# Tile 0's P is transposed at place 7 of a pair, in front of the other pair's second P V group

## The reference, cut to what matters

```
scale = 1.0 / np.sqrt(q.shape[-1])
scores = scale * np.matmul(q, k.transpose(0, 1, 3, 2))       # 4 x 8 heads, 576 x 576, depth 64
thresh = np.max(scores, axis=-1, keepdims=True) - tau
scores = np.where(scores >= thresh, scores, -1000000000.0)
scores = scores - np.max(scores, axis=-1, keepdims=True)
attn = np.exp(scores)
attn = attn / (np.sum(attn, axis=-1, keepdims=True) + 1e-09)
x = np.matmul(attn, v)                                       # -> 2304 tokens x 512
...
h = x @ w_in;  r = np.maximum(h, 0.0);  x = (s * (r * r) + b) @ w_out
...
h = x @ w_in2; x = (np.maximum(h, 0.0) + alpha * np.minimum(h, 0.0)) @ w_out2
```

## Time and profile before

| what | value |
| --- | --- |
| time, median of 3 runs | 1088.46 us (1088.38 to 1089.14) |
| time of the profiled execution | 1089.1 us |
| its span | 1087.3 us |
| TensorE busy | 99% of the span |
| VectorE, ScalarE, GpSimd busy | 48%, 47%, 24% of the span |
| mean granted TensorE clock | 0.996 of full speed |
| one pair in the steady part of attention | 17.34 us |

### The profile page before, as it was taken

One profiled execution on the slowest core, in us unless ns is written; L12 is line 12 of the kernel. 1 busy time (PEld: TensorE's weight loads), 2 busy tenths in 40 slices (PEclk: granted clock), 3 DMA queues, 4 the chain that ended last, 5 costly groups with the idle time before them and its releaser, 6 DMA issues.

```text
span 1087.3 us, 18967 instructions
## 1 busy us (share of the span) xinstructions
PE 1075.3 (99%) x5826; PEld 892.6 (82%) x5826; DVE 526.4 (48%) x1017; ACT 505.9 (47%) x946; POOL 257.3 (24%) x438
## 2 busy tenths in 40 slices
PE   8999999999999999999999999999999999999998
PEld 7877877777788888888888889888888888888897
DVE  7988989888643332242242246522422332332232
ACT  4877878787754332232232235544433333333343
POOL 3666656666574200000000014322000000000000
PEclk8999999999999999999999999999999999999999
DMA  8666666565121100000000003211100100010010
GB/s 187 159 148 160 153 143 157 139 152 135 40 58 49 49 1 1 1 0 0 0 0 0 0 20 88 87 49 30 40 0 0 39 0 0 0 39 0 0 39 20
DMA packets 86554, 59.28 MB, mean 55 GB/s; under 512 B 49376, under 2 KB 69872, under 8 KB 86512
## 3 DMA queue, kind: packets, MB, share of 16 engines
q1 hardware_dynamic: 83248, 57.58, 20.6%
q10 hardware_dynamic: 3264, 1.18, 0.5%
HBM read 30.94 MB, written 4.72 MB: 33 GB/s over the span
## 4 chain that ended last, share of the span: by engine, by line
PE 91%; ACT 3%; DVE 2%; issue 2%; SPq 1%; DMA 0%; ACTq 0%; DVEq 0%
PE psum L947 23%; PE psum L948 23%; PE psum L949 23%; PE psum L1084 6%; PE psum L1050 5%; PE psum L976 3%; PE psum L978 3%; DVE act_r L883 2%; PE psum L1079 1%; ACT pt L645 1%; PE psum L960 1%; PE psum L1058 1%; ACT ex L623 1%; ACT win_hi L600 1%; SPq L434 1%
## 5 line engine op out<-in xcount | busy, mean ns | idle before, releaser
L947 PE MATMUL psum<-x_hi,win_hi 128*128 128x512 f32 (+1 forms) x640 | 235.7, 368 | 0.0
L948 PE MATMUL psum<-x_lo,win_hi 128*128 128x512 f32 (+1 forms) x640 | 235.5, 368 | 0.0
L949 PE MATMUL psum<-x_hi,win_lo 128*128 128x512 f32 (+1 forms) x640 | 235.5, 368 | 0.0
L947 PEld LDWEIGHTS psum<-x_hi,win_hi 128*128 128x128 f32 x640 | 120.7, 189 | 20.8 <-DVE x_lo L876 0.2
L948 PEld LDWEIGHTS psum<-x_lo,win_hi 128*128 128x128 f32 x640 | 120.6, 188 | 20.4
L949 PEld LDWEIGHTS psum<-x_hi,win_lo 128*128 128x128 f32 x640 | 120.7, 189 | 19.9
L894 DVE SCALAR_TENSOR_TENSOR act_r<-act_n,nalpha,act_r 128x512 f32<-128x512 f32 (+1 forms) x80 | 56.1, 702 | 155.6 <-ACT act_r L724 155.4
L883 DVE SCALAR_TENSOR_TENSOR act_r<-act_r,s_c 128x512 f32<-128x512 f32 (+1 forms) x80 | 73.1, 914 | 111.0 <-ACT act_r L713 111.0
L716 ACT ACTIVATE g_hi<-act_r,b_c 128x512 fp32r<-128x512 f32 (+1 forms) x80 | 54.5, 681 | 151.7 <-PE psum L949 121.6
L557 POOL TENSOR_SCALAR ex<-ex,none_in,rinv 128x576 f32<-128x576 f32 x142 | 117.1, 827 | 30.0 <-DVE rinv L814 29.2
L623 ACT ACTIVATE ex<-psum,negm 128x576 f32<-128x576 f32 x144 | 107.1, 747 | 29.2 <-DVE negm L795 28.1
(11 more groups left out here) (94 smaller groups left out, 1611.2 us busy)
## 6 DMA issues: line engine op xcount, KB each, us to landing
k_twice<-k_hi SPq DMA_DIRECT2D x64, 144.0 KB, 2.4
stage<-in_moe_w_out_dram SPq DMA_DIRECT2D x32, 256.0 KB, 2.6
out_dram<-stage SPq DMA_DIRECT2D x18, 256.0 KB, 2.2
q_both<-q_hi SPq DMA_DIRECT2D x32, 128.0 KB, 2.3
q_both<-q_lo SPq DMA_DIRECT2D x32, 128.0 KB, 2.3
win_raw<-in_moe_w_in_dram SPq DMA_DIRECT2D x16, 256.0 KB, 2.9
stage<-in_moe_w_in_dram SPq DMA_DIRECT2D x16, 256.0 KB, 2.7
raw_q<-in_q_dram SPq DMA_DIRECT2D x30, 128.0 KB, 2.4
```

The source lines that it names most:

```text
L947: nc.tensor.matmul(dst, lhs[0], rhs[0], start=first, stop=False)
L948: nc.tensor.matmul(dst, lhs[0], rhs[1], start=False, stop=False)
L949: return nc.tensor.matmul(dst, lhs[1], rhs[0], start=False, stop=final)
```

## The change

Turn 0 goes from place 8 to place 7 in the table. At place 8 it stood behind the other pair's second P V group and behind the fill of tile 7; now it stands in front of both.

```
@@ -212,7 +212,7 @@
-        TURNS = [(8, 0, False), (9, 1, False), (10, 2, False), (10, 3, False), (11, 0, True),
+        TURNS = [(7, 0, False), (9, 1, False), (10, 2, False), (10, 3, False), (11, 0, True),
                  (11, 4, False), (12, 5, False), (13, 6, False), (13, 7, False), (16, 4, True)]
```

## The result

| kernel | median us | lowest to highest | runs | span of the profiled execution | its own time |
|---|---|---|---|---|---|
| before | 1088.78 | 1087.92 to 1089.43 | 20 | 1087.3 | 1089.10 |
| changed | 1090.26 | 1089.91 to 1092.12 | 20 | 1088.6 | 1090.37 |

The ratio is 1.0017, with an interval of 1.0011 to 1.0023: 0.17% slower, inside the band of 0.2% that was forecast as the likeliest, and inside the range; the upper end of the interval lies outside the band. It is nevertheless a real loss of some 1.8 us where 0.0 was worked out, and the trace says where it lies.

A forecast was written before the change was run, and what follows sets the result against it. The prediction took a ring over four engines, no single one, as the bound. +0.3 us over 15 pairs and -0.3 in pair 0 summed to 0.0, giving a median of 1088.5 us, range 1086.2 to 1091.0.

The forecast's parts named there:

- the band of 0.2%: Whole kernel: time within 0.2% (2.2 us) of before, about what a measurement can tell from no change; chance 0.63.
- +0.3 - 0.3 = 0.0: Whole kernel, in us: +0.02 a pair over 15 pairs, less 0.3 gained in pair 0, leaves the time unchanged.
- Turn 1's wait: TensorE behind the fill of tile 8: the wait for ScalarE's copy of group 1 goes, freeing 0.14 us.
- Turn 0's slot: TensorE between the fill of tile 6 and P V: four transposes take 0.44 us, bounds 0.35 and 0.50.
- VectorE and ScalarE: Steady pair: tile 7's maximum 0.44 us later, tile 8's 0.23 later, ScalarE's exponential of tile 8 0.07 earlier.
- The mask of tile 8: VectorE: start set by the latest of ScalarE 165.16, VectorE 165.27, GpSimd 165.25, against 165.23; +0.02 us a pair taken.
- the ring: Chain of waits over four engines, from tile 7's fill through tile 8's mask and turn 8 back, 17.34 us a pair.
- GpSimd's queue decides: Rival: tile 8's threshold, queued behind tile 4's normalising, delays the mask; +0.22 us a pair, 1091.5 us, chance 0.14.
- Nothing absorbs it: Rival: an engine lacks the slack read, so the whole 0.44 us a pair goes round; 1095.1 us, chance 0.05.
- the bank wait decides: Rival: VectorE and GpSimd keep up with turn 1's earlier copy, winning up to 0.14 us a pair; 1085.8, chance 0.18.
- What would show it: Signs in a steady pair's profile; wrong if threshold releases mask after long idle, turn 1 waits, or pair moves over 0.15.
- Pair 0, -0.3: First pair, no P V beside it: turn 0 moves into TensorE's 0.62 us idle; 0.3 us gained, between 0 and 0.62.

The follow-up runs named there:

- the banks alone: The kernel before with only the two banks and their waits handed out as in the changed kernel, turn 0 left at place 8; 1086.65 us, ratio 0.9984.
- the place by itself: The changed kernel with the two banks handed out as before, turn 0 kept at place 7; 1090.92 us, ratio 1.0023.
- the kernel before with the guard twice: The kernel before with GpSimd's guard instruction of tiles 6 and 7 written twice, the extra one into a spare tile; 1088.64 us, ratio 1.0004.
- the kernel before without guards: The kernel before with GpSimd's guard for fully masked rows left out and none_in set to 0 once; 1085.05 us, ratio 0.9969.

## Why the prediction was right, and where it wasn't

**The range and the band** held, but the sum did not: it said +0.3 - 0.3 = 0.0, and the medians moved by +1.5 us (+1.8 by the ratio). Two terms cancelled in the forecast that did not cancel on the chip. That the outcome still fell in the band is in part luck: 0.17% against a limit of 0.2%, from a mechanism that the sum had not priced.

**Turn 1's wait, 0.14 to be had:** right, and measured by itself, 0.14 at the mask and 0.12 a pair.

**Turn 0's slot, 0.44:** right, 0.45. The gap in front of P V did not go under it, as the lower bound had allowed. The estimate from the Trainium skill, TensorE: Matmul & The Clock Gate, Back-to-back issue gap, of 81 ns for each transpose, would have made it 0.32; the trace of the changed kernel does not agree, with 0.45 / 4 = 112 ns each.

**VectorE and ScalarE:** maximum of tile 7 +0.44, of tile 8 +0.23, exponential of tile 8 earlier by 0.10 where 0.07 was worked out. Right.

**The mask of tile 8:** +0.02 was taken and +0.06 measured. The path that decided is VectorE's own, which was priced at 165.27, that is +0.04; of three paths the latest decides, but the sum took the 165.25 of GpSimd's path. The other 0.02 lies in the idle of 0.19 that was read as slack: 0.05 of it stays, as the gap between VectorE's sum (182.80 to 182.96) and the mask, while the way from tile 8's maximum to that sum is 0.03 shorter (1.50 us instead of 1.53). GpSimd's threshold for the mask, whose news was bounded by 0 and 0.34, ended at 182.78, 0.23 before the mask. It was not the release: with the banks alone it had ended 0.47 before the mask (180.09 to 180.56), and there too the mask stands 0.21 behind the start of the sum. So the hand-over from GpSimd to VectorE is at most 0.23.

**The step that failed** is the one that costed nothing behind the mask. The prediction says that GpSimd "had idled 0.56 us when it normalises tile 6", and reads the ring from there as following the mask one to one. Of the 0.56, 0.31 is the hand-over from the guard in front of it, which a normalising pays in all these rows when the guard that it needs stands right in front of it; the slack was 165.56 + 0.22 + 0.31 to 166.34 = 0.25 in that pair (guard at 165.56 in the trace before) and 0.31 in the next. The same section had worked out that the normalising of tile 4 is delayed by the full 0.44 and followed the queue to the threshold of tile 8, but not the two instructions further to the guard. There 0.43 meets 0.31: 0.12 a pair lost, where the mask alone, late by 0.06, would have lost 0.06.

**The rival "GpSimd's queue decides"** had the right engine, the right cause (tile 4's normalising, reached in full) and the right sign, at the wrong instruction: by the guard of tiles 6 and 7 and not by tile 8's threshold. The 0.145 a pair are 2.2 us, two thirds of the 3.3 that it put on the pairs. "Nothing absorbs it" and "the bank wait decides" are refuted by the table of steps; the second is what the banks alone do.

**What would show it:** P V 0.44 later, an idle of 0.9, turn 1 right behind the fill and the mask within 0.1 all came. The pair at 17.3 to 17.4 did not: 17.49, a movement of 0.145, just under the 0.15 that was to refute the forecast.

**Pair 0, -0.3:** at the full clock this term has no ground. The two idles that it was worked out from the earlier trace rows stand in a stretch of the profiled execution in which the granted clock was 0.50 (shown in the last section). At the full clock, VectorE's maxima of tiles 7 and 8 in pair 0 read so, with the banks alone (turn 0 at place 8) and then in the changed kernel (place 7):

```profile
22.28 0.75 DVE L795 TENSOR_REDUCE negm<-psum 128x1 f32<-128x576 f32 x1
...
23.82 0.74 DVE L795 TENSOR_REDUCE negm<-psum 128x1 f32<-128x576 f32 x1
```

```profile
22.46 0.75 DVE L795 TENSOR_REDUCE negm<-psum 128x1 f32<-128x576 f32 x1
...
24.00 0.74 DVE L795 TENSOR_REDUCE negm<-psum 128x1 f32<-128x576 f32 x1
```

It is 1.54 us in both, and neither waits for TensorE: VectorE bounds pair 0 there, and the place of turn 0 changes nothing between them. So the forecast's balance of +0.3 and -0.3 was luck; without this term it would have been +0.3. That 15 x 0.145 = 2.2 is more than the 1.8 measured is no sign of a gain in pair 0. It can come from the clock, as the last section says.

## What to carry to other kernels

An idle in front of an instruction that waits for two things is not all slack: subtract the hand-over of the other wait, here 0.31 of 0.56, before anything is hidden in it. When a fill is made late, follow its delay down the slowest queue to the last instruction before the next wait that is far off, and not only to the one that the argument was about. And where one number in a table sets both the place of work and the order of banks, try them apart; here the banks by themselves gained 0.12 a pair, the place by itself lost 0.14, and together they lost 0.145. Last, before an idle is priced, look at the granted clock of the stretch that it stands in.

## What the runs showed of the hardware

**A hand-over within one engine.** The hand-over of 0.31 us stands between two instructions of the same engine, GpSimd, in each kernel where the guard decides. News from VectorE to GpSimd took 0.21 (166.13 to 166.34, kernel before).

**The clock in the opening.** The profiled execution of the kernel before had a stretch at the lower clock level, which the changed one's had not. The columns of these rows are the stretch, its length, busy us (instructions) of PE, PEld, DVE, ACT and POOL, the granted clock, DMA share and GB/s; before first, then changed.

```profile
18.00:20.00 2.00, 2.00 (x11) 2.00 (x10) 1.09 (x2) 0.50 (x1) 1.14 (x3) 0.50 1.13 277
20.00:22.00 2.00, 1.38 (x6) 1.03 (x6) 2.00 (x5) 1.12 (x3) 0.99 (x2) 0.50 0.55 120
```

```profile
18.00:20.00 2.00, 1.88 (x14) 1.64 (x14) 1.84 (x4) 0.59 (x1) 1.60 (x4) 1.00 0.98 284
20.00:22.00 2.00, 1.26 (x9) 0.79 (x7) 1.98 (x5) 1.52 (x4) 1.21 (x3) 1.00 0.69 152
```

0.50 is 1.2 GHz, 1.00 is 2.4 GHz. Ahead of the fall TensorE had stood idle for 2.02 us, waiting for a DMA of k_twice; ahead of the changed kernel's 18 us it had idled 1.35. The idle alone doesn't decide it: at the same place the kernel before with the guard twice idled 1.77 us and fell to 0.50, and the kernel before without guards idled 1.80 us and stayed at 1.00. What brings the fall in some executions is open. Runs without a trace show only their mean clock; if one of 0.997 means such a stretch, it costs about 1 us: of the 23 runs of before timed beside the banks alone, the five with a mean clock of 0.997 have a median of 1089.27, the thirteen at 1.0 one of 1088.28.

This bears on the result. Ten of the 20 runs of before stand at 1089.0 us or above, where its profiled execution with that stretch also lies (1089.1), and none of the 20 runs of the changed kernel had a mean clock under 0.998. So the median of before may hold a part of this 1 us, and the change may cost somewhat more than 1.5 to 1.8 us, nearer to the 2.2 of the pairs. The clocks of most of those 20 runs are not on record, so this is not shown.
